# Gate fold spread singly among the tiles of turns 0 and 1, an own bank for y of chunk 1, last sums in two parts, compares in halves with idle products in search 2

## The chip, the cores and the metric

The kernel runs on one core of a Trainium2 chip. The time is device microseconds of one execution. Engines are named as in the profile: PE is TensorE (PEld its weight loads), DVE is VectorE, ACT is ScalarE, POOL is GpSimd, SP is SyncE, whose queue issues most DMAs.

## The reference, cut to what matters

Three stages follow each other, all in float32:

```python
# attention with a decaying state: B, H, S, D = 4, 8, 768, 48
for t in range(S):
    cur = einsum('bhd,bhe->bhde', u[None] * kt, vt)
    y[:, :, t] = einsum('bhd,bhde->bhe', rt, state + cur)
    state = wt[..., None] * state + einsum('bhd,bhe->bhde', kt, vt)
# x = y as 3072 rows of 384
h = x @ w_in                      # 384 -> 2048
g = h * tanh(log1p(exp(h)))
x = g @ w_out                     # 2048 -> 384
# experts, each with room for 384 of the 3072 rows
logits = x @ w_gate               # 8 experts
# the (row, expert) pairs in order of falling logit: a row goes to the first
# expert in its order that is not yet full
for e in range(8):
    out[mask] = maximum(x[mask] @ w1[e], 0) @ w2[e]
```

## The kernel before, in words

**Tiling.** The 3072 rows are 24 chunks of 128 rows. Two chunks make a turn (`CH = 2`), so there are 12 turns. Matrix products run as three float16 products: high part by high part, low by high, high by low. Every engine has its own program, a list in order written out by hand; semaphores join them. What stands ahead of what is fixed by the `turn(i, slot)` functions, 16 slots to a turn.

**The attention of a chunk n.** DVE makes the running product of the decays (`products`), its reciprocal in two parts (`inverse`), `kdiv` (`key_side`, L926) and `rdec` (`query_side`, L933). PE makes the scores (`scores`), DVE masks them (`masks`, into `att`), PE turns kdiv (`keys`) and makes y into a PSUM bank and the state's increment into another (`values`, L440). POOL makes the diagonal products r*k*u (`diagonal`) and dv (`own`), with the dot products of DVE (`dots`) between the two. DVE adds y and dv (`sum_x`, L955), PE turns x (`turn_x`, L467) into the bank of y, ACT rounds it to `x_hi`, DVE makes `x_lo` from it. y of every chunk is in bank 7 (`Y`); `values(n)` therefore waits for x_hi and x_lo of the chunk before. The first two chunks run ahead of turn 0, with idle products (`warm`) on PE in between.

**A turn's slots.** In slots 0 to 7 PE runs the 8 tiles of x @ w_in (`tile(i, j)`, 18 products of 128x256 each, into three banks in rotation). Tile j >= 3 waits for DVE's copy of tile j - 2 (`copied`, L988, semaphore `hcp`), so tile (1,3) waits for the copy of tile (1,0). In slots 8 to 15 PE runs `sums(i - 1, j)`, 12 products of 128x392 each, of the turn before, into banks 0 and 1; turn 0 has none. ACT does tanh and arctan in slots 0 to 8, the sines at slot 8, and rounds g afterwards; DVE multiplies (`gated`, L995) in slots 9 to 15, ahead of the copies of the next turn. The attention of later chunks is laid between the slots; in turn 0 that of chunks 2 and 3, in slots 3 to 7.

**The gate fold.** w_out @ w_gate is made once on PE: 16 column groups of three float32 products of 128x8 each, 48 in all, into bank 0. From there ACT and DVE put it beside w_out as 8 more columns (392 instead of 384), so that the sums give the logits too; these two copies, `foldhi` and `foldlo`, stand in slot 4 of ACT and slot 6 of DVE in turn 1, and `sums(0, 0)` waits for them. The fold runs in four blocks of 12 products: after tile (0,3), at the end of slot 7 of turn 0, and in slots 1 and 2 of turn 1. Its turned weights lie in the buffers of g_hi and g_lo (first two quarters) and in two of their own.

**The end of the first stage.** After the last turn PE makes only the logits of its two chunks (`last_logits`), then two of their eight sums. The other six are laid into search 1.

**The searches.** Expert by expert (7 searches, r = 0 to 6) a threshold is searched in 6 steps of 32 limits. A step: DVE compares 24 columns of keys with 32 limits (`compare`, L1209, 128x768), PE counts (`counts`, 24 products of 8 columns), DVE tests `full`, PE spreads it (`maxima`), DVE reduces it (`most`) and makes the next limits. After 6 steps `choose` names the expert and its rows, `ranks` numbers them, the next search starts. The experts' products are laid between: for expert p, X turns the gathered rows, H0 to H7 are the first product (9 products of 128x384), Y0 to Y7 the second. In search 1 no expert is ready; behind the maxima of each step stands one of the six late sums. In search 2 (r = 1) PE has only units I and J (the row numbers of the first expert, for the gather by POOL), then X in step 4, H0 and H1 in step 5, and H2, Y0, H3 after it. From search 3 on PE is full. Units are placed by this table:

```python
PLACES = {("A", 0): ["Y1"], ("B", 0): ["H4"], ("A", 1): ["I", "Y2"], ("B", 1): ["J", "H5"],
          ("A", 2): ["Y3"], ("B", 2): ["H6"], ("A", 3): ["Y4"], ("B", 3): ["H7"],
          ("A", 4): ["Y5"], ("B", 4): ["X", "Y6"], ("A", 5): ["Y7"],
          ("B", 5): ["H0", "H1"], ("C", 0): ["H2", "Y0", "H3"]}
```

All matrix products are recorded at L413 (the helper `mm`), all activations at L726, so they are told apart by their operands: fold products read `w_gate`, scores `rdec,kdiv`, idle products `ident` alone, counts `oh,cmp`, maxima `full`. A float32 product of PE has two records. The start of PE's program, where `values(1)` stands between `keys(1)` and `turn_x(1)`, is L594 to L611; the searches on PE begin at L617.

Of the kernel before, what the change touches and what calls it, by code (L numbers as in the profile page):

```python
# [13 lines left out]
P = 128  # L14
# [45 lines left out]
def moe_chain(nc, wt_d, kt_d, rt_d, r_d, k_d, v_d, u_d, win_d, wout_d, wg_d, wot_d, w1_d, w2_d, out_d):  # L60
# [4 lines left out]
    with ctx:  # L65
# [3 lines left out]
        def sem(name):  # L69
# [129 lines left out]
                 "oh", "cmp", "cnt", "full", "np", "mem", "rank", "numbered", "one_hot", "copies", "idblk", "blocks", "idps", "ids", "maxin", "maxout", "rd",  # L199
# [41 lines left out]
        STEPS = 2  # L241

# [168 lines left out]
        def _(pe):  # L411
# [28 lines left out]
            def values(n):  # L440
# [4 lines left out]
                pe.wait_ge(s["xhi"], n)  # L445
                pe.wait_ge(s["xlo"], n)
                pe.wait_ge(ld["v"][c], 16 * (n // CH + 1))
                for q in range(NQ):
                    if not first_of(n):
                        mm(Y[:, 2 * q * D:(2 * q + 2) * D], rdec[c][:, q, :], state[:, q, :], start=True, stop=False)  # L450
                    for h in (2 * q, 2 * q + 1):
                        last = mm(Y[:, h * D:(h + 1) * D], att[:, h, :], v_tok[c][:, h, :],
                                  start=first_of(n), stop=first_of(n) or h % 2 == 1)
# [9 lines left out]
            def turn_x(n):  # L463
                c = n % CH
                pe.wait_ge(s["x"], n + 1)
                for k3 in range(KT):
                    last = nc.tensor.transpose(Y[:, k3 * P:(k3 + 1) * P], x_tok[c][:, k3 * P:(k3 + 1) * P],  # L467
                                               ident[:, :])
                last.then_inc(s["xT"], 1)

            def tile(i, j):
# [13 lines left out]
                elif i == 0:  # L485
                    pe.wait_ge(s["att"], 4)
                for f in range(2):
# [28 lines left out]
            def sums(i, j):  # L516
# [9 lines left out]
                rounded_parts(i, j)  # L526
                for c in range(CH):
                    for f in range(2):
                        t = (2 * j + f) * TOK + c * P
                        hi_, lo_ = g_hi[:, t:t + P], g_lo[:, t:t + P]  # L530
                        first, end = j == 0 and f == 0, j == NJ - 1 and f == 1
                        mm(ab[c][:, 0:DE], hi_, wout_hi[:, 2 * j + f, :], start=first, stop=False)
                        mm(ab[c][:, 0:DE], hi_, wout_lo[:, 2 * j + f, :], start=False, stop=False)
                        last = mm(ab[c][:, 0:DE], lo_, wout_hi[:, 2 * j + f, :], start=False, stop=end)
                last.then_inc(s["mm"], 1)
# [3 lines left out]

            def folded(qs):  # L540
                pe.wait_ge(s["gload"], 16)
# [1036 lines left out]
```

## Time and profile before

| | us |
|---|---|
| median of 3 runs | 848.12 |
| lowest, highest | 845.80, 849.88 |
| the profiled execution: its time | 849.38 |
| the profiled execution: its span | 847.6 |
| PE busy in it | 802.7 |
| DVE busy in it | 641.2 |
| ACT busy in it | 405.4 |
| POOL busy in it | 282.4 |

The span is the time from the first to the last instruction of the profiled execution; all instants below count from its start. The mean granted clock of PE is 0.968 of full speed. Busy PE includes the modelled ends of pipelined products, so it hides short gaps. The stages by time: the first two chunks up to 30 us, turn 0 to 67, turn 1 with the sums of turn 0 to about 118, the other turns to 556, search 1 to 587, search 2 to 614, five more searches with the experts, then the last experts alone.

### The profile page before, as it was taken

Reading aid. Unit: us, or ns where it says so; the run is one execution under the profiler, and the core shown is the slowest. Engines: PE = TensorE matmul, PEld = TensorE weight load, DVE = VectorE, ACT = ScalarE, POOL = GpSimd, SP = SyncE. Lnnn points to the kernel's source line nnn. Section 1 sums busy time; section 2 is a strip of 40 time slices with the busy share of each in tenths; the row PEclk is TensorE's granted clock in tenths of the full one; section 3 lists DMA queues with packets and bytes.
Section 4 is the critical chain, followed back from the end, with each engine's and each line's share of the span. In section 5 each row is a group of like instructions: output and inputs, shape, how many; then the busy total and the mean of one; then the engine's idle time right before and its main releaser. Section 6 shows DMA issues by size and latency. Waiting matters only on the chain. (4 is left out here: it accounts for less than half of the span.)

```text
span 847.6 us, 16953 instructions
## 1 busy us (share of the span) xinstructions
PE 802.7 (95%) x6744; PEld 596.4 (70%) x6744; DVE 641.2 (76%) x1123; ACT 405.4 (48%) x655; POOL 282.4 (33%) x244
## 2 busy tenths in 40 slices
PE   8999999999999999999898999986799999999995
PEld 8888878787878787868676777754465665666662
DVE  8879788898979897979696987767768677776220
ACT  2457557575767667575756476920112211212221
POOL 3315262534444443444251625001212312313311
PEclk9897999999999999999999999998599999999999
DMA  9952236363545445463817354103324244235410
GB/s 312 334 193 61 72 125 249 105 243 125 218 155 201 173 168 207 140 232 120 315 59 289 121 182 136 75 20 131 139 106 177 68 167 178 89 146 205 190 43 29
DMA packets 47790, 133.48 MB, mean 157 GB/s; under 512 B 5344, under 2 KB 19808, under 8 KB 45664
## 3 DMA queue, kind: packets, MB, share of 16 engines
q1 hardware_dynamic: 38880, 93.07, 31.2%
q0 software_dynamic: 5376, 34.61, 11.1%
q10 hardware_dynamic: 3456, 4.72, 1.5%
q8 instruction: 54, 0.88, 0.4%
q14 instruction: 24, 0.20, 0.1%
HBM read 97.78 MB, written 34.60 MB: 156 GB/s over the span
## 5 line engine op out<-in xcount | busy, mean ns | idle before, releaser
L413 PE MATMUL bank<-x_hi,win_hi 128*128 128x256 f16 x576 | 160.5, 279 | 0.0
L413 PE MATMUL bank<-x_lo,win_hi 128*128 128x256 f16 x576 | 160.3, 278 | 0.0
L413 PE MATMUL bank<-x_hi,win_lo 128*128 128x256 f16 x576 | 160.1, 278 | 0.0
L1438 POOL TENSOR_TENSOR g_lo<-t_sb,g_hi 128x512 f16<-128x512 f32 x88 | 117.4, 1355 | 82.0 <-ACT g_hi L726 82.0
L413 PE MATMUL bank<-wout_hi,g_hi 128*128 128x392 f16 (+1 forms) x416 | 129.5, 318 | 0.8 <-issue 0.8
L413 PE MATMUL bank<-wout_lo,g_hi 128*128 128x392 f16 (+1 forms) x416 | 129.2, 317 | 0.0
L413 PE MATMUL bank<-wout_hi,g_lo 128*128 128x392 f16 (+1 forms) x416 | 129.1, 317 | 0.0
L1422 POOL TENSOR_TENSOR dv<-v_tok,dot 128x384 f32<-128x384 f32 x24 | 39.6, 1649 | 210.3 <-DVE dot L948 210.3
L726 ACT ACTIVATE g_lo<-bank 128x384 f16<-128x384 f32 x64 | 31.4, 490 | 144.5 <-PE bank L413 144.5
L726 ACT ACTIVATE g_hi<-t_sb 128x512 f16<-128x512 f32 x96 | 56.8, 624 | 89.1 <-DVE t_sb L995 65.9
L995 DVE TENSOR_TENSOR t_sb<-t_sb,h_sb 128x512 f32<-128x512 f32 x96 | 89.8, 964 | 5.4 <-ACT t_sb L726 3.4
L726 ACT ACTIVATE t_sb<-h_sb 128x512 f32<-128x512 f32 x96 | 60.1, 626 | 64.5 <-DVE h_sb L988 64.4
L918 DVE RECIPROCAL inv<-cum 128x256 f32<-128x256 f32 x48 | 83.3, 1737 | 0.0
L988 DVE TENSOR_SCALAR h_sb<-bank 128x512 f32<-128x512 f32 x96 | 64.0, 667 | 15.9 <-PE bank L413 15.9
L726 ACT ACTIVATE t_sb<-t_sb,half 128x512 f32<-128x512 f32 x96 | 67.1, 706 | 0.0
L1309 DVE SCALAR_TENSOR_TENSOR g_lo<-bank,g_lo 128x384 f16<-128x384 f32 x64 | 35.1, 549 | 41.0 <-ACT g_lo L726 40.6
L413 PEld LDWEIGHTS bank<-x_hi,win_hi 128*128 128x128 f16 x576 | 58.3, 101 | 9.3 <-issue 0.2
L413 PEld LDWEIGHTS bank<-x_lo,win_hi 128*128 128x128 f16 x576 | 57.5, 100 | 7.9
L413 PEld LDWEIGHTS bank<-x_hi,win_lo 128*128 128x128 f16 x576 | 57.6, 100 | 7.7
L726 ACT ACTIVATE stage<-stage 128x1536 f16<-128x1536 f32 (+1 forms) x33 | 48.6, 1473 | 25.5 <-DMA stage<-in_moe_w 25.5
L726 ACT ACTIVATE t_sb<-t_sb,half_pi 128x512 f32<-128x512 f32 x96 | 60.7, 709 | 0.1
L413 PEld LDWEIGHTS bank<-wout_hi,g_lo 128*128 128x128 f16 x416 | 40.1, 98 | 26.4 <-issue 0.3
(179 smaller groups left out, 1514.0 us busy)
## 6 DMA issues: line engine op xcount, KB each, us to landing
stage<-in_moe_w SPq DMA_DIRECT2D x32, 768.0 KB, 6.7
w_split<-stage SPq DMA_DIRECT2D x32, 768.0 KB, 5.3
wt<-in_w_turned SPq DMA_DIRECT2D x24, 258.0 KB, 5.3
kt<-in_k_turned SPq DMA_DIRECT2D x24, 256.0 KB, 4.8
rt<-in_r_turned SPq DMA_DIRECT2D x24, 256.0 KB, 5.2
r_tok<-in_r SPq DMA_DIRECT2D x24, 192.0 KB, 6.5
k_tok<-in_k SPq DMA_DIRECT2D x24, 192.0 KB, 6.8
v_tok<-in_v SPq DMA_DIRECT2D x24, 192.0 KB, 4.8
```

Of the source, the lines that this page charges most:

```text
L413: return nc.tensor.matmul(*a, **k)
L726: return nc.scalar.activation(out, in_, f, **k)
L918: V.reciprocal(inv[:, qs, :], cum[n % CH][:, qs, 1:PW]).then_inc(s["inv"], 1)
L988: V.tensor_scalar(h_sb[:, j * GW:(j + 1) * GW], hb[HB[j]][:, :], 0.5, None, ALU.mult).then_inc(s["hcp"], 1)
L995: V.tensor_tensor(t, t, h_sb[:, j * GW:(j + 1) * GW], ALU.mult).then_inc(s["g"], 1)
L1309: V.scalar_tensor_tensor(h_lo[f % 3][:, :], bank[3 + f % 3][:, 0:CAP], 0.0, h_hi[f % 3][:, :], ALU.max, ALU.subtract).then_inc(s["hlo"], 1)
L1422: G.tensor_tensor(dv[:, :, :], v_tok[c][:, :, :], dot[:, :].rearrange("p (h o) -> p h o", o=1).to_broadcast([P, H, D]), ALU.mult).then_inc ...
L1438: G.tensor_tensor(g_lo[:, j * GW:(j + 1) * GW], t_sb[:, j * GW:(j + 1) * GW], g_hi[:, j * GW:(j + 1) * GW], ALU.subtract).then_inc(s["glo" ...
```

## The change

Five edits, of which the diff shows the core. (1) y, its turned x and their readers use bank 1 for chunk 1 alone, and the values of chunk 1 no longer wait for x_hi and x_lo of chunk 0; three idle products stand ahead of them. POOL waits for rdec of chunk 1 before its diagonal. (2) The 48 fold products are issued one at a time behind every third product of a tile: six in each of tiles 4 to 7 of turn 0, four in each of tiles 0 to 5 of turn 1; the wait for their weights stands ahead of tile (0,4). ACT's copy of the gate columns moves from slot 4 to 6, DVE's from 6 to 7. (3) Of each of the six late sums in search 1, 3 of 12 products now stand ahead of the maxima and 9 behind. (4) In searches 1 and 2 the compare is two instructions of half the columns, and the counts begin on the first half. (5) In search 2 PE gets idle products (float32, 128 columns, into a bank not in use): 14 before it, 4 after the first counts, 5 after each of the maxima of steps 0 to 3. 

```diff
+        def y_bank(n):
+            return ab[1] if n == 1 else Y
...
                 pe.wait_ge(s["att"], 2 * n + 2)
                 if not first_of(n):
                     pe.wait_ge(s["state"], with_keys(n))
-                pe.wait_ge(s["xhi"], n)
-                pe.wait_ge(s["xlo"], n)
+                if n > 1:
+                    pe.wait_ge(s["xhi"], n)
+                    pe.wait_ge(s["xlo"], n)
                 pe.wait_ge(ld["v"][c], 16 * (n // CH + 1))
...
+            to_fold = [(t, k3) for t in range(FT) for k3 in range(KT)]
+            FOLDS = {**{(0, j): 6 for j in range(4, NJ)}, **{(1, j): 4 for j in range(6)}}
+
+            def fold_one():
+                t, k3 = to_fold.pop(0)
+                q, f = t // (FT // 4), t % (FT // 4)
+                last = mm(ab[0][:, t * E:(t + 1) * E], wot[q][:, k3, f * P:(f + 1) * P], w_gate[:, k3, :],
+                          start=k3 == 0, stop=k3 == KT - 1)
+                if f == FT // 4 - 1 and k3 == KT - 1:
+                    last.then_inc(s["fold"], 1)
...
+                folds = FOLDS.get((i, j), 0)
+                if (i, j) == (0, 4):
+                    pe.wait_ge(s["gload"], 16)
+                    pe.wait_ge(s["wotload"], 64)
...
                         last = mm(hb[HB[j]][:, f * TOK:(f + 1) * TOK], a, b, start=t == 0, stop=t == len(ops) - 1)
+                        if folds and t % 3 == 1 and 3 * f + t // 3 < folds:
+                            fold_one()
...
                     if slot == 3:
-                        folded([0])
                         scores(2)
...
                         turn_x(3)
-                        folded([1])
...
-                if i == 1 and slot in (1, 2):
-                    folded([slot + 1])
...
             keys(1)
+            warm(ident[:, :], 3)
             values(1)
...
-                pe.wait_ge(s["cmp"], NSTEP * r + t + 1)
+                if r < 2:
+                    pe.wait_ge(s["cmp_half"], NSTEP * r + t + 1)
+                else:
+                    pe.wait_ge(s["cmp"], NSTEP * r + t + 1)
                 for j in range(NT):
+                    if r < 2 and j == NT // 2:
+                        pe.wait_ge(s["cmp"], NSTEP * r + t + 1)
                     last = mm(R[0:NTHR, 0:E], cmp[:, j, :], oh[:, j, :], start=j == 0, stop=j == NT - 1)
...
+            def idle_products(n):
+                for _ in range(n):
+                    mm(yb[2][:, 0:P], ident[:, :], ident[:, :], start=True, stop=True)
+
             for r in range(E - 1):
+                if r == 1:
+                    idle_products(14)
                 for t in range(NSTEP):
                     counts(r, t)
+                    if r == 1 and t == 0:
+                        idle_products(4)
                     units(r, ("A", t), unit)
+                    if r == 0:
+                        sums(NI - 1, SUMS["B", t], slice(0, 3))
                     maxima(r, t)
+                    if r == 1 and t < 4:
+                        idle_products(5)
                     units(r, ("B", t), unit)
                     if r == 0:
-                        sums(NI - 1, SUMS["B", t])
+                        sums(NI - 1, SUMS["B", t], slice(3, None))
...
-                if i == 1 and slot == 4:
+                if i == 1 and slot == 6:
                     act.wait_ge(s["fold"], 4)
...
-                    if i == 1 and slot == 6:
+                    if i == 1 and slot == 7:
                         dve.wait_ge(s["foldhi"], 1)
...
+            def compare(x, limits, parts):
+                n = NT // parts
+                for h in range(parts):
+                    x_part = x[:, h * n:(h + 1) * n].rearrange("p (j o) -> p j o", o=1).to_broadcast([P, n, NTHR])
+                    ins = V.tensor_tensor(cmp[:, h * n:(h + 1) * n, :], x_part,
+                                          limits[:, :].rearrange("p (o i) -> p o i", o=1).to_broadcast([P, n, NTHR]),
+                                          ALU.is_ge)
+                    ins.then_inc(s["cmp" if h == parts - 1 else "cmp_half"], 1)
...
             own(0)
+            pool.wait_ge(s["rdec"], 2)
             diagonal(1)
             own(1)
```

## Rows read from the trace of the kernel before

**Rows 1.** Table of stretches; PEclk is the granted clock, each engine busy us (xcount).

```profile
24.60:31.40 6.80, 6.80 (x35) 6.30 (x34) 4.51 (x8) 3.34 (x3) 2.24 (x3) 0.50 1.03 413
...
41.70:45.10 3.40, 3.40 (x21) 2.81 (x20) 2.83 (x4) 3.25 (x5) 0.00 (x0) 0.50 0.77 246
...
65.60:86.00 20.40, 20.40 (x129) 16.54 (x128) 17.83 (x18) 14.33 (x23) 12.58 (x10) 0.67 0.18 53
...
588.00:600.00 12.00, 4.43 (x107) 3.65 (x107) 9.33 (x32) 0.00 (x0) 2.97 (x3) 0.50 0.69 272
```

**Rows 2.** Timeline, PE, start of the kernel: start, us, engine, line, operation, idle before.

```profile
15.53 2.87 PE L413 MATMUL bank<-ident 128*128 128x128 f32 x24
...
22.30 0.43 PE L413 MATMUL bank<-state,rdec 128*128 128x96 f32 x2 [0.94 <-DVE x_lo L981]
...
29.88 0.42 PE L413 MATMUL bank<-x_hi,win_hi 128*128 128x256 f16 x1
```

**Rows 3.** Timeline, POOL and DVE, chunk 1 ahead of turn 0.

```profile
16.73 1.34 POOL L1415 TENSOR_TENSOR ruk<-ruk,u_b 128x384 f32<-128x384 f32 x1
...
17.12 1.49 DVE L933 TENSOR_TENSOR rdec<-rt,cum 128x512 f32<-128x512 f32 x1
...
25.56 0.56 DVE L955 TENSOR_TENSOR x_tok<-bank,dv 128x384 f32<-128x384 f32 x1 [1.40 <-PE bank L413]
```

**Rows 4.** Timeline, PE, turn 0: a fold block, tile (0,6) to what follows it, scores.

```profile
38.50 2.74 PE L413 MATMUL bank<-w_gate,g_hi 128*128 128x8 f32 x24
...
52.32 0.27 PE L413 MATMUL bank<-x_hi,win_hi 128*128 128x256 f16 x1
...
54.29 0.49 PE L467 MATMUL bank<-ident,x_tok 128*128 128x128 f32 x3
...
55.43 1.68 PE L413 MATMUL bank<-rdec,kdiv 64*128 64x128 f32 x16 [0.65 <-DVE kdiv L926]
```

**Rows 5.** Timeline, DVE, turns 0 and 1.

```profile
38.00 0.69 DVE L933 TENSOR_TENSOR rdec<-rt,cum 128x512 f32<-128x512 f32 x1
...
62.46 0.56 DVE L955 TENSOR_TENSOR x_tok<-bank,dv 128x384 f32<-128x384 f32 x1 [0.51 <-PE bank L413]
...
67.01 3.76 DVE L995 TENSOR_TENSOR t_sb<-t_sb,h_sb 128x512 f32<-128x512 f32 x6 [1.43 <-ACT t_sb L726]
...
78.22 0.68 DVE L988 TENSOR_SCALAR h_sb<-bank 128x512 f32<-128x512 f32 x1
```

**Rows 6.** Timeline, DVE and PE, searches 1 and 2.

```profile
566.20 0.96 DVE L1209 TENSOR_TENSOR cmp<-key,thr 128x768 bf16<-128x768 f32 x1
...
565.51 0.17 PE L413 MATMUL bank<-full,rest_b 32*128 32x8 bf16 x1 [0.68 <-DVE full L1219]
...
567.71 0.76 PE L413 MATMUL bank<-oh,cmp 128*32 128x8 bf16 x24
...
568.78 0.17 PE L413 MATMUL bank<-full,rest_b 32*128 32x8 bf16 x1 [0.32 <-DVE full L1219]
...
588.40 0.78 PE L413 MATMUL bank<-oh,cmp 128*32 128x8 bf16 x24 [4.00 <-DVE cmp L1209]
...
588.59 0.46 DVE L1281 TENSOR_TENSOR t_sb<-high,iota_hi 128x288 f16<-128x288 f32 x1
...
592.25 0.80 PE L413 MATMUL bank<-oh,cmp 128*32 128x8 bf16 x24 [1.54 <-DVE cmp L1209]
...
595.10 0.80 PE L413 MATMUL bank<-oh,cmp 128*32 128x8 bf16 x24 [1.10 <-DVE cmp L1209]
...
595.96 0.17 DVE L1303 TENSOR_SCALAR ids<-row_no 128x3 uint32<-128x3 f32 x1
```

**Rows 7.** Timeline, PE, end of search 2 and first counts of search 3.

```profile
602.28 2.18 PE L659 MATMUL bank<-ident,h_sb 128*128 128x128 f32 x9 [0.17 <-DMA h_sb<-x_rows,ids]
...
605.81 5.94 PE L413 MATMUL bank<-g_hi,win_hi 128*128 128x384 f16 x18
...
616.15 0.76 PE L413 MATMUL bank<-oh,cmp 128*32 128x8 bf16 x24
```

More of the change, by code:

```diff
@@ L198, in moe_chain @@
                  "phi", "plo",
-                 "oh", "cmp", "cnt", "full", "np", "mem", "rank", "numbered", "one_hot", "copies", "idblk", "blocks", "idps", "ids", "maxin", "maxout", "rd",
+                 "oh", "cmp", "cmp_half", "cnt", "full", "np", "mem", "rank", "numbered", "one_hot", "copies", "idblk", "blocks", "idps", "ids", "maxin", "maxout", "rd",
                  "wrow", "xg", "xgT", "xgThi", "xgTlo", "hh", "hhi", "hlo", "m2", "ylast", "y", "yout"]
@@ L514, in last_logits, with sums @@
                 last.then_inc(s["logit"], 1)
-            def sums(i, j):
+            def sums(i, j, part=slice(0, None)):
                 if i == 0 and j % 2 == 0:
@@ L526, in sums @@
                 rounded_parts(i, j)
+                ops = []
                 for c in range(CH):
@@ L530, in sums @@
                         hi_, lo_ = g_hi[:, t:t + P], g_lo[:, t:t + P]
+                        w_hi, w_lo = wout_hi[:, 2 * j + f, :], wout_lo[:, 2 * j + f, :]
                         first, end = j == 0 and f == 0, j == NJ - 1 and f == 1
[L532 to L535, printed above, removed]
+                        ops += [(c, hi_, w_hi, first, False), (c, hi_, w_lo, False, False), (c, lo_, w_hi, False, end)]
+                for c, g, w, start, stop in ops[part]:
+                    last = mm(ab[c][:, 0:DE], g, w, start=start, stop=stop)
+                if part.stop is None:
+                    last.then_inc(s["mm"], 1)
             def finish(i, step):
                 pass
-            def folded(qs):
-                pe.wait_ge(s["gload"], 16)
-                pe.wait_ge(s["wotload"], 64)
-                for q in qs:
-                    for f in range(FT // 4):
-                        t = q * FT // 4 + f
-                        for k3 in range(KT):
-                            last = mm(ab[0][:, t * E:(t + 1) * E], wot[q][:, k3, f * P:(f + 1) * P], w_gate[:, k3, :],
-                                      start=k3 == 0, stop=k3 == KT - 1)
-                    last.then_inc(s["fold"], 1)
             def turn(i, slot):
@@ L1227, in next_step @@
                                                 ALU.mult, ALU.add))
-                    compare(key, thr)
+                    compare(key, thr, 2 if r < 2 else 1)
                     link(V.scalar_tensor_tensor(lo[t + 1][:, :], m, w, lo[t][:, :], ALU.mult, ALU.add))
@@ L1236, in next_step @@
                     link(V.tensor_scalar(res[:, :], near[:, :], lo[t + 1][:, 0:1], None, ALU.subtract))
-                    compare(res, grid[NSTEP - 1])
+                    compare(res, grid[NSTEP - 1], 2 if r < 2 else 1)
             def weight_row(r, x):
@@ L1368, in _ @@
                 if r < E - 2:
-                    start_search()
+                    start_search(r + 1)
                     digits()
```

23 lines of the change are left out of this document (10 added, 13 removed).

## The prediction

> **What bounds the kernel now.** I began with the page: TensorE is busy for 802.7 of 847.6 us, so time can only come from its idle stretches, its half-clock stretches and its work. The table of stretches then shows where the clock falls [rows 1]: 0.50 is the level of 1.2 GHz, 1.00 that of 2.4 GHz. It is 0.50 from 24.6 to 31.4 us, from 41.7 to 45.1, on average 0.67 from 65.6 to 86.0 (three spells, 13.5 us at half), 0.50 from 588 to 600, and the products that follow run at that pace too [rows 7]. These are the stretches that the change touches. The timelines say what lay ahead of each fall: at the start a wait and narrow float32 products [rows 2]; in turns 0 and 1 a block of gate folds [rows 4]; in search 2 an almost idle TensorE [rows 6]. Between turn 2 and the end of the sums TensorE has no gap that the edits touch, so I let every microsecond won before it arrive at the end.
>
> **The start.** Chunk 1's values wait 0.94 us for x_lo of chunk 0 [rows 2]. With a bank of its own for y that goes, and three idle products stand there, at 2.87 / 12 = 0.24 us each [rows 2]. The new POOL wait keeps diagonal(1) off VectorE's rdec(1), which took 1.49 us where rdec(2) takes 0.69 [rows 3, 5], while POOL's product ran beside it (16.73 to 18.07) [rows 3]. diagonal(1) then ends near 20.2 instead of 18.1; who waits for it is dots(1), queued behind masks(1), which even in the new order end near 20.8, so the wait costs nothing. Without that cover it costs up to 2.1. scores(1) can start 0.4 us earlier (the 12 idle products ahead of it end at 18.4), y of chunk 1 is done near 24.0, and with TensorE busy throughout I expect full clock there. sum_x(1) then waits for dv(1) (near 24.3), no longer 1.40 us for TensorE [rows 3], and tile (0,0) starts near 27.15 instead of 29.88 [rows 2], at full clock. VectorE's queue (products, split, copies, reciprocals) then ends rdec(2) at 35.6 instead of 38.7 [rows 5]. **Gain 3.1 us.**
>
> **Turn 0 from there.** A tile is 54.29 - 52.32 = 1.97 us; a fold in its block is 2.74 / 12 = 0.22 us, its two weight loads being longer than its 8 columns [rows 4]. Interleaved, a fold costs from 0 (hidden) to about 0.33 (its 0.22 and one more exposed load); I take 0.22, the nearest row. Today rdec(2) to the end of y of chunk 3 is 62.4 - 38.7 = 23.7 us [rows 5]. Afterwards: scores 1.65, a wait of 0.65 for the split of weight piece 2, tiles 4 to 7 with six folds each 4 x (1.97 + 1.34) = 13.2, keys twice 1.0, values(2) 3.6, turn_x 0.45, scores(3) 1.65, y(3) 2.6: 24.8 us. The wait for the gate's weights moves from ahead of 38.50, where it holds up nothing [rows 4], to about 37.9: 0 to 0.6 us, and I take 0. No DMA is moved. The block of 12 after tile 3 and the half clock behind it go, but the second block, which lay behind y(3), now lies ahead of it. **Loss 1.1 us, net gain 2.0.** By bounds of the fold: gain 4.6 or 0.
>
> The Trainium skill, "TensorE: Matmul & The Clock Gate", Step-by-step: what each phase is for, says that weight loads are pulled ahead of running matmuls into the background buffer. By that rule one of a fold's two loads lies under the 256-column product, a fold costs 0.11, and turn 0 would win 2.7 us more.
>
> **Turn 1.** ScalarE's sines and VectorE's gating set the next date: gated products from 67.01 after a wait for ScalarE, then reciprocals, kdiv, rdec, and the copy of tile (1,0) only at 78.22 [rows 5]; tile (1,3) waits for that copy. All this moves up by 2.0, to 76.9. TensorE, at full clock and without blocks, is through tiles 0 to 2 at about 72 (start 63.5, three times 1.97 + 0.88) and idles some 5 us. So most of the 6.7 us that the half clock cost from 65.6 to 86.0 is not won: the stretch turns VectorE-bound. Idle for 4.00 us before 588.40 was followed by half clock [rows 1, 6], so tile (1,3) starts at half clock again. Tile 3 at half clock takes 4.9, scores 1.65, tiles 4 and 5 with their folds 5.7, keys 0.5, tile 6 1.97, values(4) 3.6, tile 7 1.97: 76.9 + 20.3 = 97.2, less 0.4 for what is back at full clock within it, instead of today's 99.5. If the clock holds all along, VectorE's queue sets it, and it is 94.5. The later gate copies (slots 6 and 7) put a wait of up to 1.6 us before sum_x(4), which stands in for one of 1.4 us for TensorE; turn_x(4) comes a tile later, so I cost it at nothing; without that tile it would be 0.5. **Gain up to here 2.7 (2.3 to 5.0).**
>
> **Search 1.** A step is 568.78 - 565.51 = 3.27 us and bound by TensorE: counts 0.76, a wait of 0.32 for `full`, the maxima 0.1, and the 12 sums with the rest, 2.1 [rows 6]. Three sums (0.5 us) now fill that wait and delay the maxima by 0.19, nine stay behind: a step becomes some 2.9 instead of 3.27. Five steps win 0.4 each, 2.0 (1.5 if the sums' own 0.31 is all). The compare in halves lengthens VectorE: 384 elements cost 0.56 us by the line through 288 (0.46) and 768 (0.96) [rows 6], and instructions start 0.08 before the last ends, so 0.08 more each, behind TensorE here except at the first (-0.1). The later maxima before choose costs 0.2, which leaves 1.7. **Gain 1.8**, since the maxima of the first step, where `full` waits for VectorE, move by nothing.
>
> **Search 2.** A step is 595.10 - 592.25 = 2.85 us and VectorE-bound: TensorE waits 1.54 us for the compare [rows 6], then 24 counts. With halves, 12 counts lie under the second half; won 0.38 a step at full clock, none below half that. What matters is the ids at 595.96 [rows 6], two steps in: gather and transposes (which ended their wait on the gather, [rows 7]) start about 2.2 us earlier in all. The 14 idle products (3.3 us at full clock) fit before 588.40, where TensorE waits 4.00 us [rows 6]; the 4 fit before `full`; 5 after the maxima (1.2 us) end as the first half compare does (566.20 - 565.51 = 0.69 from maxima to compare, and its 0.56, [rows 6]). They cost nothing at full clock. Their cover is gone at half clock, where five take 5 x 0.47 = 2.35 us.
>
> The H products behind the transposes ran from 605.81 at half clock, 18 in 5.94 us, and counts of search 3 started at 616.15 [rows 7]. If the clock holds all through, up to 3.0 us come back there and 0.6 in the transposes. But TensorE idles again before the gather lands and before H0, so I take half, 1.5. **Gain of both searches 1.8 + 0.4 + 1.5 = 3.7 (2 to 5.8).**
>
> The Trainium skill, "VectorE: DVE Perf Modes", The TRN2 errata, gives a fixed term of about 150 cycles for each instruction, an estimate of 0.16 us. By that rule each split compare costs 0.16 and not the 0.08 of my line, and the searches win 0.5 us less.
>
> **Sum.** 2.7 + 3.7 = 6.4. The profiled execution took 849.4 us (span 847.6), the median of the runs is 848.1: 843.0 on the first, 841.7 on the second. I forecast 841.7, by the median.
>
> **Rivals.** (A) Forecast, 839 to 843.9: 0.50. (B) The clock holds where I let it fall (tile (1,3), H0): 5.0 + 5.8 = 10.8, 837.3 to 839. For: TensorE keeps far busier; against: both idle stretches stay. 0.20. (C) The idle products don't hold the clock in search 2. A step is then 0.10 + 2.35 + 0.07 + 0.76 + 0.37 = 3.65 instead of 2.85, four cost 3.2, the transposes start 0.9 late: searches lose 0.9 in place of 3.7 won, 848.1 - 2.7 + 0.9 = 846.3. For: the counts between them are only 8 columns wide. Against: float32 products of 128 columns held the clock at the start. 0.12. (D) The start keeps its half-clock spell, or VectorE's queue eats the win in turns 0 and 1: turns give 0.5 to 1.0, 843.5 to 844. 0.12. (E) **Slower:** the folds, a third of the time of their tiles, pull the clock down for whole tiles as the blocks did. Tiles 4 to 7 of turn 0 then take 13.2 us more, tiles 3 to 5 of turn 1 some 5 more beyond the cover: 848 + 18 - 6 = 860. It decides at tile (0,4), where the granted clock would be 0.50. Against: two thirds of each tile stay 256 columns wide. 0.06.
>
> **Numbers.** About 0.5% (4.2 us) is what a measurement of this kernel can tell from no change; the bound is 843.9. Faster is A, B and half of D: 0.76. Same is C and half of D: 0.18. Slower is E: 0.06. The range 837 to 846.5 holds B to C and leaves out E, and the chance that several terms err the same way.
>
> **What would show it.** Right: clock 1.00 from 24 to 31 and 41 to 66; first product of a tile near 27; singles of 8 columns between products of 256, spaced 0.22 more; TensorE idle 4 to 5 us before tile (1,3), waiting for `h_sb`; search 1 steps of 2.9; search 2 steps of 2.5 and ids near 593.8 less the turns' 2.7. Wrong: half clock in a tile with folds; folds spaced beyond 0.33; tile (1,3) without a wait; search 2 steps above 2.85.

## The result, and the profile after

The changed kernel took 852.33 us (median of 6 runs, 850.13 to 852.88) against 848.04 (6 runs, 845.61 to 849.88) of the kernel before on the same chip: a ratio of 1.004, 95% interval 1.0021 to 1.0059. The forecast was 841.7, in a range of 837 to 846.5. A second measurement with more runs, `after_again` below, is 1.0025. The change is a small loss, and the prediction was wrong in size and sign. The profiled execution took 852.56 us, its span is 850.8 (before 847.6).

The ledger below has the start of the same VectorE or TensorE work in the two profiled executions (`late` is a VectorE instruction that stands once, at the end of a search).

| | before | after | difference |
|---|---|---|---|
| tile (0,0), first product | 29.88 | 27.90 | -1.98 |
| rdec(2) | 38.00 | 38.64 | +0.64 |
| x_tok(3), end of turn 0 | 62.46 | 65.01 | +2.55 |
| x_tok(4), turn 1 | 96.77 | 98.51 | +1.74 |
| x_tok(5) | 110.32 | 111.08 | +0.76 |
| `full` of search 1, first step | 565.29 | 566.21 | +0.92 |
| `late`, end of search 1 | 582.24 | 582.04 | -0.20 |
| `late`, end of search 2 | 606.12 | 609.93 | +3.81 |
| `late`, end of search 3 | 639.82 | 643.05 | +3.23 |

In these two executions, then, two things went wrong: between 28 and 39 us the whole gain of the start is lost, and search 2 costs 4.0 us. From search 3 on the two run in step.

One execution stands for each side, and the kernel before varies much by itself, since its half clock does not always fall in the same place. `searchonly`, an experiment below, is the kernel before up to search 1, and its profile has x_tok(5) 4.20 us earlier than the 110.32 of the ledger:

```profile
106.12 0.56 DVE L965 TENSOR_TENSOR x_tok<-bank,dv 128x384 f32<-128x384 f32 x1 [0.36 <-PE bank L413]
```

`beforewait`, the kernel before with one more wait, has it at 108.11. A difference of some 4 us up to search 1 in such a ledger is thus no gain or loss of a kernel; the medians decide that.

**28 to 39 us.** The timelines of VectorE and GpSimd of the changed kernel (start, us, engine, line, operation, idle before):

```profile
27.53 1.44 DVE L940 TENSOR_TENSOR_SCAN cum<-wt,heads 128x516 f32<-128x516 f32 x1
28.89 4.64 DVE L1038 SCALAR_TENSOR_TENSOR win_lo<-stage,win_hi 128x1536 f16<-128x1536 f32 x1
33.46 0.68 DVE L1019 TENSOR_SCALAR h_sb<-bank 128x512 f32<-128x512 f32 x1
...
38.64 0.68 DVE L964 TENSOR_TENSOR rdec<-rt,cum 128x512 f32<-128x512 f32 x1
```

```profile
28.83 3.09 POOL L1466 TENSOR_TENSOR win_lo<-stage,win_hi 128x1536 f16<-128x1536 f32 x1 [0.95 <-ACT win_hi L757]
```

VectorE's split of a weight piece took 4.64 us. The same kind of split takes 1.75 at 21.64 in this profile. GpSimd's split of another piece had begun 0.06 us earlier; it ended at 28.83 + 3.09 = 31.92, and VectorE's ended 1.61 later, about its own length. VectorE's queue is 2.9 us late from there, and TensorE with it:

```profile
27.90 0.27 PE L416 MATMUL bank<-x_hi,win_hi 128*128 128x256 f16 x1 [1.44 <-DVE x_lo L1012]
...
33.64 0.27 PE L416 MATMUL bank<-x_hi,win_hi 128*128 128x256 f16 x1 [1.65 <-issue]
...
39.42 1.75 PE L416 MATMUL bank<-rdec,kdiv 64*128 64x128 f32 x16 [1.70 <-DVE kdiv L957]
```

Tile (0,0) does start 1.98 us earlier, but two waits of 1.65 and 1.70 us follow which the kernel before does not have there, and half clock comes after them, just where the tiles carry their folds. The table of stretches (us, then each engine's busy time, then PEclk) shows this and the other half-clock stretches:

```profile
24.60:31.40 6.80, 5.36 (x48) 4.66 (x48) 6.61 (x8) 3.35 (x3) 4.62 (x3) 1.00 1.04 409
40.90:47.60 6.70, 6.19 (x36) 5.14 (x36) 4.50 (x7) 3.75 (x5) 2.48 (x3) 0.50 0.70 237
68.40:71.70 3.30, 3.30 (x22) 2.85 (x21) 2.26 (x4) 3.29 (x6) 0.00 (x0) 0.51 0.05 18
81.90:85.90 4.00, 4.00 (x24) 3.18 (x23) 4.00 (x5) 1.58 (x4) 4.00 (x3) 0.58 0.43 132
...
590.70:609.00 18.30, 16.50 (x180) 14.74 (x180) 11.24 (x40) 1.47 (x3) 3.16 (x3) 0.50 0.36 136
```

The first row answers to the first of [rows 1]: full clock at the start, as forecast. But 6.7 us at half in turn 0 stand where 3.4 were. The last row lies within a stretch at half from 590.4 to 614.3; in the kernel before it was from 587.8 to 611.7, as long. So the idle products did not hold the clock here, they only stood in a stretch that was at half before too.

**The folds.** TensorE in tile (0,6), a fold after each third product, and what follows the tile:

```profile
54.09 0.27 PE L416 MATMUL bank<-x_hi,win_hi 128*128 128x256 f16 x1
54.20 0.27 PE L416 MATMUL bank<-x_lo,win_hi 128*128 128x256 f16 x1
54.31 0.29 PE L416 MATMUL bank<-w_gate,g_lo 128*128 128x8 f32 x2
54.45 0.27 PE L416 MATMUL bank<-x_hi,win_lo 128*128 128x256 f16 x1
...
56.89 0.49 PE L472 MATMUL bank<-ident,x_tok 128*128 128x128 f32 x3
```

The tile is 56.89 - 54.09 = 2.80 us instead of 1.97 [rows 4], so six folds cost 0.83, **0.14 apiece**; in a block they cost 0.22.

**Turn 1 and search 2.** TensorE ahead of tile (1,3), and in search 2:

```profile
81.37 0.28 PE L416 MATMUL bank<-x_hi,win_hi 128*128 128x256 f16 x1 [3.93 <-DVE h_sb L1019]
...
590.53 2.50 PE L416 MATMUL bank<-ident 128*128 128x128 f32 x10
592.96 0.80 PE L416 MATMUL bank<-oh,cmp 128*32 128x8 bf16 x24
...
597.84 2.50 PE L416 MATMUL bank<-ident 128*128 128x128 f32 x10
600.27 0.80 PE L416 MATMUL bank<-oh,cmp 128*32 128x8 bf16 x24
...
609.62 5.40 PE L416 MATMUL bank<-g_hi,win_hi 128*128 128x384 f16 x18
```

Five idle products take 2.50 us at half clock, and the counts stand behind them without a wait: VectorE's compares are done 0.8 us before them (at 592.14 for the counts at 592.96). A step takes 3.67 us (590.21 to 593.88 by `full`), the next 3.63, 4.58 and 3.67, where they took 2.83 to 2.88 before [rows 6]. In the step of 4.58 VectorE's `full` also started 0.9 us later after the counts than in the others, which the profile before has nowhere (see Open).

### The profile page after: what moved, and what is told of

Same layout as the page of the kernel before. It is cut to its first block and busy times, and to the rows that moved or that the text cites. A ratio compares the mean times of both kernels' runs of the same rounds, so it can differ in the third digit from the quotient of the medians.

```text
span 850.8 us, 17130 instructions
## 1 busy us (share of the span) xinstructions
PE 809.4 (95%) x6826; PEld 602.4 (71%) x6826; DVE 644.6 (76%) x1135; ACT 405.6 (48%) x655; POOL 281.1 (33%) x244
## 5 line engine op out<-in xcount | busy, mean ns | idle before, releaser
L757 ACT ACTIVATE g_lo<-bank 128x384 f16<-128x384 f32 x64 | 31.4, 491 | 143.9 <-PE bank L416 138.7
L1026 DVE TENSOR_TENSOR t_sb<-t_sb,h_sb 128x512 f32<-128x512 f32 x96 | 90.4, 971 | 5.4 <-ACT t_sb L757 3.4
L416 PEld LDWEIGHTS bank<-x_hi,win_lo 128*128 128x128 f16 x576 | 62.0, 108 | 6.0
```

Source lines behind the costliest of these rows:

```text
L416: return nc.tensor.matmul(*a, **k)
L757: return nc.scalar.activation(out, in_, f, **k)
L1026: V.tensor_tensor(t, t, h_sb[:, j * GW:(j + 1) * GW], ALU.mult).then_inc(s["g"], 1)
```

## The experiments

Each ratio is to the kernel before, run beside it on the same chip. Its own median moved from chip to chip (848.23, 849.25, 846.05 and 846.02 us), so ratios are compared, and medians only where both kernels ran on one chip.

### The two suspects: `poolwait`, `noidle`, `both`, `foldonly`

`poolwait` makes GpSimd's splits wait until VectorE's second split of this kind is done; `noidle` takes out the idle products of search 2; `both` does both.

```diff
             def split_scaled(n):
                 pool.wait_ge(s["whi"], n + 1)
+                pool.wait_ge(s["wlo"], 2)
...
             for r in range(E - 1):
-                if r == 1:
-                    idle_products(14)
...
-                    if r == 1 and t == 0:
-                        idle_products(4)
...
-                    if r == 1 and t < 4:
-                        idle_products(5)
```

`foldonly` is the kernel before with the second edit alone: folds spread, gate copies later.

> The changed kernel plus one wait: POOL's win_lo (weight piece 3) waits until VectorE's split of piece 1 is done. Theory P (the win at the start is lost because POOL's product started at 28.83, 0.06 us before VectorE's split, which then took 4.64 us instead of 1.73): VectorE's split takes 1.7 again, rdec of chunk 2 ends near 36.4 instead of 39.3, the first masks and x_tok of turns 0 and 1 come 2.5 to 3 us earlier, and the whole is 2 to 3 us faster than the changed kernel, near 849.5. Rival (the stretch is bound elsewhere, by the fold or by weights from HBM): no more than 0.5 us comes back.

> The changed kernel without the 14, 4 and 5 idle products of search 2; all else kept. Theory I (the idle products fell to half clock and stood in front of the counts): the steps of search 2 go back to 2.6 to 2.85 us, search 2 loses nothing against the kernel before, the whole is 4 to 5 us faster than the changed kernel, near 847.5. Rival (the loss in search 2 comes from the halves): steps stay near 3.7 and nothing comes back.

> The POOL wait and no idle products together. If both theories hold and the two add, 6.5 to 8 us faster than the changed kernel: near 845, 3 us faster than the kernel before. If one hides the other, less than 5.

> The kernel before with the fold spread alone (and the later gate copies that go with it). Own theory (fold costs 0.14 us apiece between wide products and keeps the clock; turn 1 is VectorE-bound all the same): 1 to 2 us faster than the kernel before, near 846.5, with an idle wait of some 4 us ahead of tile (1,3). Rival (the spread fold is itself what costs 0.8 us by turn 2): 0.5 to 1.5 us slower.

| | median, us (range, runs) | ratio, 95% |
|---|---|---|
| poolwait | 848.36 (845.31 to 854.31, 12) | 1.0005, 0.9981 to 1.0029 |
| noidle | 849.96 (847.41 to 855.16) | 1.0031, 1.0011 to 1.005 |
| both | 845.67 (843.54 to 849.8) | 0.9973, 0.9954 to 0.9992 |
| foldonly | 851.69 (846.85 to 856.28, and one of 2777.86) | 1.0033, 1.0007 to 1.0059 |

**The splits.** VectorE's and GpSimd's split in `noidle`, in `poolwait` and in `foldonly`, a fence for each view:

```profile
29.16 1.73 DVE L1032 SCALAR_TENSOR_TENSOR win_lo<-stage,win_hi 128x1536 f16<-128x1536 f32 x1
```

```profile
29.32 4.53 POOL L1460 TENSOR_TENSOR win_lo<-stage,win_hi 128x1536 f16<-128x1536 f32 x1 [2.02 <-ACT win_hi L751]
```

```profile
29.34 1.73 DVE L1038 SCALAR_TENSOR_TENSOR win_lo<-stage,win_hi 128x1536 f16<-128x1536 f32 x1
```

```profile
31.21 3.10 POOL L1467 TENSOR_TENSOR win_lo<-stage,win_hi 128x1536 f16<-128x1536 f32 x1 [3.74 <-DVE win_lo L1038]
```

```profile
29.45 4.65 DVE L1009 SCALAR_TENSOR_TENSOR win_lo<-stage,win_hi 128x1536 f16<-128x1536 f32 x1
```

```profile
29.39 3.10 POOL L1432 TENSOR_TENSOR win_lo<-stage,win_hi 128x1536 f16<-128x1536 f32 x1 [1.81 <-ACT win_hi L728]
```

Whoever starts first takes its own time, and the other's ends one full length behind it: in `noidle` 29.16 + 1.73 = 30.89, and GpSimd's ends at 33.85, 2.96 later. In `foldonly`, which has the old start, GpSimd was first by 0.06 us. Of the eight profiled executions of this study without the added wait VectorE's split took 4.6 us in four (the changed kernel in all three of its profiles, and `foldonly`). In the other four it took 1.7 and GpSimd's 3.7 to 4.6. The Trainium skill, "SBUF — State Buffer", Who interferes with whom, says that a VectorE instruction with two SBUF inputs contends with a GpSimd instruction that reads SBUF, that the shared pair of ports is locked by one of them, and that the order of issue decides who blocks. Every one of these rows agrees. With the wait, x_tok(2) starts at 49.34 in `poolwait` instead of 53.36.

**Search 2.** In `poolwait` the same code had full clock until 602.4 us and its steps took 2.56, 2.93, 3.97 and 3.20; in `noidle` the clock was at half, and they took 2.59, 2.95, 3.86 and 2.60. At half clock, then, the change's idle products cost 0.7 to 1.1 us a step, 3.6 over the whole of search 2 (27.9 us against 24.3 in `noidle`). From `late` of search 1 to that of search 3 `noidle` wins 0.7 us on the kernel before, the changed kernel loses 3.4. In the medians the difference of `both` to `poolwait` is 2.7 us (the idle products; the intervals just overlap), that of `noidle` to the changed kernel's own measurement 2.4 (on another chip, 0.8 by ratios). `both` and `noidle` ran on one chip and differ in GpSimd's wait alone: 4.3 us, and the intervals lie apart. This is the test of the collision in the medians. It is more than the 3 us of one collision, and in the one profiled execution of `noidle` VectorE's split happened to come first, so what else the wait changes isn't known. Neither cause alone explains the loss; with both taken out the kernel is 0.27% faster than before, still not the 0.76% of the forecast.

### Turn 1: `bothfill`, `earlyfill`, `startonly`, `searchonly`

In `both` TensorE still idles 3.94 us ahead of tile (1,3), and half clock follows (76.8 to 80.2); in `poolwait` it lasted from 76.7 to 90.4. `bothfill` fills 3.74 us of that wait. `earlyfill` has 9 products there and the folds of turn 1 eight to a tile in tiles (1,0) to (1,2). `startonly` and `searchonly` are the kernel before with edit (1), or with (3) and (4), alone.

```diff
             def tile(i, j):
...
+                if (i, j) == (1, 3):
+                    for _ in range(16):
+                        mm(ab[1][:, 0:P], ident[:, :], ident[:, :], start=True, stop=True)
                 if j >= 3:
                     pe.wait_ge(s["hcp"], NJ * i + j - 2)
```

> The POOL wait and no idle products in search 2, plus 16 idle float32 products (3.8 us at full clock, into bank 1) ahead of tile (1,3), where TensorE waits for VectorE's copy of tile (1,0). Theory T (turn 1's half clock comes from that wait, and the folds in tiles (1,3) to (1,5) then keep it): the granted clock stays 1.00 from 66 to 100 us, x_tok of chunks 4 and 5 come at least as early as in the best profile so far (93.4 and 106.0), and the slow executions of the kernel without the fill (848 to 850) go: median 843 to 844.5. Rival (the clock falls whatever TensorE does in the wait): half clock stays, nothing gained, or up to 2 us lost because 16 products at half clock outlast the wait.

> As the last, but turn 1's 24 folds stand 8 to a tile in tiles (1,0) to (1,2), ahead of the wait, and 9 idle products fill what is left of it. Theory T: the folds cost nothing there, since TensorE would wait anyway; tiles (1,3) to (1,5) take 1.97 us each; 1 to 1.7 us faster than the kernel with 16 idle products if TensorE bounds the rest of turn 1, equal to it if VectorE does. Rival (folds belong among busy tiles): the clock falls in tiles (1,0) to (1,2), where folds take 1.1 of 3.1 us.

> The kernel before with the start's edits alone (own y bank for chunk 1, three idle products, POOL behind rdec). Theory P: the tile (0,0) starts 2 us earlier, VectorE's split of weight piece 1 meets POOL's win_lo again and takes 4.6 us in most executions, so that nothing is left by x_tok of chunk 2: within 1 us of the kernel before. Rival: the start's win stays, 2 to 3 us faster.

> The kernel before with the late sums in two parts and the compares in halves alone, no idle products. By the steps in the profiles so far: search 1 gains 1.2 us, search 2 at half clock about 0.3 net; 1 to 2 us faster than the kernel before, near 846.7. Rival (the halves cost more on VectorE than they hide): same or slower.

| | median, us (range) | ratio, 95% |
|---|---|---|
| bothfill | 843.63 (841.82 to 844.67) | 0.9938, 0.9919 to 0.9958 |
| earlyfill | 843.1 (841.98 to 846.21) | 0.9944, 0.9924 to 0.9964 |
| startonly | 847.89 (843.45 to 850.32) | 0.9986, 0.9962 to 1.0009 |
| searchonly | 846.95 (842.6 to 849.86) | 0.9976, 0.9953 to 0.9998 |

`bothfill` and `earlyfill` had full clock from 14 to 100 us, and their executions lie within 2.9 and 4.2 us of each other where those of `both` lie within 6.3: the slower executions are gone, as they would be if the clock had stayed down in these (only one execution of each was profiled). x_tok(5) is 4.57 us earlier than in the profile before in `bothfill`, 5.06 in `earlyfill`, but only 0.37 and 0.86 earlier than in `searchonly`, so the ratios and not this must carry the gain. The two do not differ in time. Against the 0.9973 of `both` the fill is worth 0.35%; by `bothfill_again` below (0.9951) it is 0.2%, with intervals that overlap. The start alone can't be told from nothing, though in its profile VectorE's split came first and took 1.7. The edits of the searches alone win 0.24%, with the upper end of the interval at 0.9998.

### The idle products of search 2: `allfill`, `hold`, and two controls

`allfill` is the changed kernel, idle products in, with the wait of GpSimd and the fill. `hold` is `earlyfill` with its idle products behind the counts, where they delay none of the step's work: 14 ahead, 7, 1, 1, 1, 1 and 4 behind the counts of the six steps, 5 behind the units of steps 0 to 3, 6 ahead of the transposes. `beforewait` is the kernel before with GpSimd's wait; `after_look` is one more execution of the changed kernel.

```diff
                     counts(r, t)
-                    if r == 1 and t == 0:
-                        idle_products(4)
+                    if r == 1:
+                        idle_products((7, 1, 1, 1, 1, 4)[t])
...
+                    if r == 1 and t == 4:
+                        idle_products(6)
                     units(r, ("B", t), unit)
```

> The changed kernel with all its idle products in search 2, the POOL wait and 16 idle products ahead of tile (1,3). The stages up to the sums are then as in the kernel with both fills and no idle products in search 2 (843.6), so the difference is the price of search 2's idle products alone. Theory I: they fall to half clock in most executions and cost 2 to 4 us: median 846 to 847.5, and executions spread more. Rival (they keep the clock more often than not when the stages before are steady): no dearer than 0.5 us, or up to 2 us faster.

> The kernel with early folds and fill (843.1), with more idle products in search 2, placed behind units I and J instead of ahead: 14 ahead of it, 7 after the first counts, 1 after those of steps 1 to 4, 5 behind the units of steps 0 to 3, 6 ahead of the transposes, 4 after the last counts. Theory H (the clock of search 2 can be held if no gap of TensorE is left, and H0 to H2 then run at full clock): granted clock 1.00 from 560 to 620, search 2 3 to 4 us shorter, median 839.5 to 840.5. Rival (the clock falls all the same and the idle products then stand in front at half clock): 3 to 5 us slower, 846 to 848.

> The kernel before with the POOL wait alone. In three other profiles with the old start TensorE kept its clock there, and POOL's win_lo and VectorE's split of piece 1 then start within 0.3 us of each other. Theory P (whoever comes second waits, and it is a toss in the kernel before too): the executions in which VectorE loses go, 0.5 to 2 us faster in the median. Rival (only the changed kernel has the meeting): no difference.

> The changed kernel once more, to see what of its profile is the kernel's and what the execution's. Theory: the meeting of POOL and VectorE at 29 us is a toss (4.6 or 1.7 us for VectorE's split), the idle wait ahead of tile (1,3) is there each time, and half clock in search 2 begins at another place. Rival: all three as in the first profile.

`allfill` 842.71 us (838.75 to 846.74), ratio 0.9957 (0.994 to 0.9973); `hold` 843.5 (841.86 to 845.01), 0.9959 (0.9945 to 0.9974); `beforewait` 846.76, 1.0002 (0.9985 to 1.0019); `after_look` 847.25 in its one execution. In `allfill` and `hold` the granted clock was 1.00 through all of search 2, and from `late` of search 1 to that of search 3 they won 3.5 and 2.4 us on the kernel before. `after_look` had it until 602.9, with steps of 2.55, 2.94, 2.54 and 2.56 us, by the same code that took 3.67, 3.63, 4.58 and 3.67. So the clock was up through the idle products' steps in some executions of this code and down in others. Of the five profiled executions that have them it fell at 590.4 us in the changed kernel's first, between 602 and 609 in three, and not at all in `allfill`; only the first was at half through the steps that hold idle products. And `allfill` keeps all five edits: with GpSimd's wait and the fill the changed kernel is 0.43% faster than the one before, so the idle products are not what makes it a loss. GpSimd's wait is worth nothing to the kernel before. `hold` had half clock from 64.1 to 81.1 us, through its tiles with eight folds; the same tiles had full clock in `earlyfill`.

### What was still open: `after_again`, `foldfill`, `best`, `bothfill_again`

`foldfill` is `foldonly` with GpSimd's wait and the fill. `best` is `bothfill` with the idle products of `hold`.

> The changed kernel once more, beside the kernel before on the same chip. Theory: its loss is made of two stretches, each of which goes one way or the other: the splits of weights near 29 us (VectorE's takes 4.6 us where GpSimd's starts first: about 2 us late up to tile (1,3), partly covered by the wait there) and search 2 (steps of 3.6 to 4.6 us if the half clock comes before its counts, 2.55 if it doesn't: 4 us). So 1.000 to 1.005 of the kernel before; in the profile, VectorE's copy near 28.9 us takes 4.6 us, and TensorE waits near 4 us before tile (1,3). Rival (the first measurement was a matter of its chip): 0.996 or less.

> The kernel before with the fold spread singly and the gate copies late, plus the wait of GpSimd's split and 16 idle products ahead of tile (1,3). Without those two it was 1.0033. Theory (the spread folds cost 0.14 us each and win only if the clock stays up through the tiles that carry them): 0.995 to 0.998, no half clock from the end of tile (1,2) to turn 2. Rival (spreading wins nothing whatever the clock does, since the folds only move): 1.000 or more.

> The changed kernel with the wait of GpSimd's split, 16 idle products ahead of tile (1,3), folds four to a tile in turn 1, and in search 2 idle products placed as in the run named hold (7, 1, 1, 1, 1, 4 behind the counts of the six steps, 6 ahead of the transposes). Theory (turn 1 with four folds a tile keeps full clock, eight a tile did not in hold; search 2 keeps it with products after the counts): 0.991 to 0.994, granted clock 1.00 from 60 to 100 us and from 585 to 615. Rival (idle products in search 2 win nothing over none): 0.994 to 0.997, as with the kernels that had none there or had them ahead of the counts.

> The run named bothfill again (wait of GpSimd's split, 16 idle products ahead of tile (1,3), none in search 2), beside the last one on the same chip, for the price of idle products in search 2 alone. Theory (they hold the clock there): bothfill is 0.5 to 2.5 us slower than the last one. Rival (they win nothing): equal within 0.5 us, near 0.994 of the kernel before.

| | median, us (range, runs) | ratio, 95% |
|---|---|---|
| after_again | 849.17 (844.44 to 853.43, and one of 2753.59; 12) | 1.0025, 1.0003 to 1.0046 |
| foldfill | 843.97 (842.48 to 846.73, 12) | 0.9965, 0.9949 to 0.998 |
| best | 841.86 (840.56 to 847.31, 12) | 0.9951, 0.9933 to 0.9969 |
| bothfill_again | 842.45 (840.64 to 844.09, 10) | 0.9951, 0.9933 to 0.9969 |

**The loss is the kernel's**, not the first chip's: 1.0025 here. Its profile has the long split again (29.44, 4.58 us) and TensorE waits 5.53 us ahead of tile (1,3), with half clock from 79.9 to 93.6 us around its end and behind it: x_tok(3) is 1.83 us later than before, x_tok(4) 4.51. In search 2 the clock held, and it won 0.8 us there.

**Spreading the folds** together with the fill and GpSimd's wait wins 0.35%, and alone (`foldonly`) it loses 0.33%: the same 48 products. The profile of `foldonly` has both troubles, the long split and a stretch at half clock from 78.2 to 88.4; that of `foldfill` has neither. The wait alone won nothing in `beforewait`; the fill was not tried without the spread folds, so what spreading by itself is worth isn't shown.

**Idle products in search 2** are worth nothing measurable: `best` and `bothfill_again` have the same ratio, though in the profiles `best` kept full clock and won 2.35 us from `late` of search 1 to that of search 3, `bothfill_again` at half clock 0.96. Two stretches of `best`, then the first product of an expert in it:

```profile
66.00:100.00 34.00, 31.14 (x287) 27.55 (x286) 31.90 (x38) 20.72 (x35) 17.87 (x13) 1.00 0.23 69
588.00:600.00 12.00, 11.72 (x169) 10.51 (x167) 9.15 (x33) 1.25 (x3) 3.03 (x3) 1.00 0.37 129
```

```profile
600.85 3.10 PE L416 MATMUL bank<-g_hi,win_hi 128*128 128x384 f16 x18
```

The 18 products of H0 and H1 take 3.10 us there against 5.40 in the changed kernel and 5.94 before [rows 7]. But `best` was 1.9 us behind `bothfill_again` when search 1 began, where the two have the same code. It had half clock from 458.1 to 461.5 and from 553.7 to 557.1 us, in the last logits (some 0.7 us of the 1.9), and `bothfill_again` had none there. The same two stretches come and go among the other profiles too; what decides it was not tried.

## Why the prediction was wrong

**The step that failed** in every profile of the changed kernel is the last one of the start: "VectorE's queue (products, split, copies, reciprocals) then ends rdec(2) at 35.6". I took that queue's durations from a profile in which GpSimd's split of 3.72 us began 0.97 us after VectorE's of 1.73, and moved VectorE's forward by 1.6 us without asking where GpSimd's would land. It landed 0.06 us ahead, and rdec(2) came at 38.64. I had even priced the same collision elsewhere, at rdec(1). rdec(2) ended at 39.3, and at 39.8 in the other two profiles. With the same start and GpSimd held back it ends at 36.3 (in `bothfill_again`) to 36.9 in seven profiles, and at 38.1 in `poolwait`, which had half clock from 28.9 to 32.3. Of the 3.7 us by which that step was wrong 2.4 to 3.0 are the collision.

**Two more steps failed with it.** "They cost nothing at full clock", of the idle products in search 2, was right as it stands, but full clock did not last: at half clock they cost 3.6 us in the first profile and nothing in the other two. And "tile (1,3) starts at half clock again" was given one tile, where it lasted up to 17 us. With GpSimd's wait and the fill added, and nothing taken out, the ratio goes from 1.0025 or 1.0040 to 0.9957 (`allfill`).

- *The start.* Full clock: right in the first profile; in `after_again`, `after_look` and `poolwait` it was at half from about 29 to 32.5. Tile (0,0) at 27.15: it came at 27.90 (its x_lo started at 27.05), and at 28.6 in the two later profiles. rdec(1) took 0.69 us instead of 1.49, as GpSimd's new wait was meant to bring. But the 3.1 us of gain were counted against an execution with half clock from 24.6 to 31.4. Of the five profiles with the old start only that one and `foldfill` have it. In `searchonly`, with the old start and full clock there, tile (0,0) came at 28.58 and rdec(2) ended at 36.9:

```profile
24.60:31.40 6.80, 5.42 (x50) 4.97 (x49) 6.07 (x9) 3.35 (x3) 3.82 (x3) 1.00 1.03 411
```

  Against such an execution a rdec(2) that ends at 36.3 wins 0.6 us, which fits `startonly`, whose gain can't be told from nothing. To take that half clock for the kernel's own was part of the error.
- *A fold costs 0.22.* It cost 0.14, between my row and the 0.11 by the rule of the Trainium skill, "TensorE: Matmul & The Clock Gate", Step-by-step: what each phase is for; 24 of them in turn 0 win 1.9 us more. (The upper bound "gain 4.6" belongs to 0.11; for a hidden fold it would be 2.0 + 24 x 0.22 = 7.3.) At half clock this is lost again: 6.7 us at half instead of none cost some 3.4 there, an estimate, behind waits that the late rdec(2) made. With neither (`bothfill`), x_tok(3) is 2.39 us earlier than in the profile before, the forecast 2.0. That is in part luck: in `searchonly` the old code has it 2.04 earlier.
- *Turn 1.* "Idles some 5 us" before tile (1,3): 3.93, right in kind, and 5.53 in `after_again`. "Starts at half clock again": right, but I let it last one tile. Seven profiles have the spread folds and no fill. In `poolwait`, `noidle` and `after_again` half clock lasted 13.7, 17.0 and 13.7 us, through tiles that carry folds, in `foldonly` 10.2, in the other three (the changed kernel's first profile, `after_look`, `both`) 3.4, 6.8 and 3.4. The four long ones stand at waits of 5.5 us and the three short ones at waits of 3.9, here `noidle` and `both`:

```profile
76.42 0.39 PE L416 MATMUL bank<-x_hi,win_hi 128*128 128x256 f16 x1 [5.54 <-DVE h_sb L1013]
```

```profile
76.25 0.28 PE L416 MATMUL bank<-x_hi,win_hi 128*128 128x256 f16 x1 [3.94 <-DVE h_sb L1013]
```

  The three short ones had 3.4 us of half clock in tiles (1,0) and (1,1) as well, so TensorE came later to a wait whose end VectorE sets. Rival E, for which I had given 0.06, had the clock down in all the tiles with folds. What the record shows is that it can stay down through them after a wait; whether the folds keep it down, or the longer wait does, isn't shown, since the same tiles came back after 3.4 us in two profiles.
- *Search 1: gain 1.8.* A step is 3.00 us, not 2.9; 1.1 won by the ledger, 1.1 to 1.3 in the other profiles with the edits. It is the one gain that every profile shows. The split compare was no part of that. In the changed kernel's timeline of VectorE both halves together take 1.02 us against 0.96 of the whole [rows 6]:

```profile
591.12 1.02 DVE L1244 TENSOR_TENSOR cmp<-key,thr 128x384 bf16<-128x384 f32 x2
```

  That is 0.06 for the split, nearer my 0.08 than the estimate of 0.16 worked out from the Trainium skill, "VectorE: DVE Perf Modes", The TRN2 errata.
- *Search 2: gain 1.9.* Lost 4.0 in the first profile, 0.9 of it from one late start of `full` that the profile before lacks; then 0.6 came back. In `after_again` and `after_look` search 2 won 0.8 and 0.9. Rival C had the mechanism and its price (3.65 us a step; 3.67, 3.63 and 3.67 measured, and one of 4.58), with a chance of 0.12. I argued that idle products had held the clock at the start; there they ran without gaps, here they stand between waits of 0.4 to 0.7 us and counts 8 columns wide.
- *Where the clock holds*, in `best`, the searches won 3.7 us on the profile before. That is the forecast's figure, but by luck: the forecast took half of what full clock should give, and by its terms for a clock that holds throughout it was 5.8. x_tok(5) came 4.58 us earlier where those terms gave 5.0, but 4.20 of it are seen in `searchonly` without the edits. In the medians `best` won 0.49%, not 0.76%.

The rivals were weighed one at a time. C and D came together in the first profile, as nothing kept them apart: each is a cover (TensorE without a gap, GpSimd behind VectorE) that the sum assumed. By the ledger the turns lost 0.9 up to search 1 where 2.7 were to be won, and the searches lost 2.3 where 3.7 were to be won: 3.6 and 6.0 of the 9.6 us between the forecast for the profiled execution (843.0) and its 852.6.

**Open.** In step 3 of searches 2 to 7 VectorE's `full` started 0.9 to 1.5 us after the counts had ended, where 0.1 is usual. This was so in the changed kernel's first profile and in every kernel profiled on two of the chips, and in none on the two others or in the profile before; it is part of the 4.58 among the steps. The kernel before had a median of 848.2 and 849.3 us on the first two chips and of 846.0 on the others, but that this is the reason was not tested. What decides whether the clock falls at a given place in one execution and not in the next stayed open. Nor was it found why one execution each of `foldonly` and `after_again` took over 2750 us.

## What to carry to other kernels

When a change moves one engine's queue forward, lay the other engines' long instructions beside it at their new times: here the 0.06 us by which GpSimd's split came first cost VectorE's 2.9. An order that matters should be a semaphore, not a lead of 1 us. Narrow products between wide ones won here only together with a filled wait ahead of them, so look for that wait. Five idle products took 1.38 us at full clock (`after_look`, at 589.53) and 2.50 at half, and delayed what stood behind them, so place them where they delay nothing. And when a gain is a stretch of half clock that goes away, profile the old kernel more than once first: here that stretch was in two profiles of five.

## What was not expected of the hardware

- A float32 product of 8 columns with its two weight loads takes 0.14 us between products of 256 columns, against 0.22 among its own kind.
- At tiles with four products of 8 columns among 18 of 256 TensorE stayed at 1.2 GHz for 10.2 to 17.0 us around and behind a wait of 5.5 us in four profiles, while the same tiles came back after 3.4 to 6.8 us in the three profiles with a wait of 3.9. With 16 idle products of 128 columns (3.74 us) in the wait the level stayed at 2.4 GHz from there to turn 2 in `bothfill`, `bothfill_again`, `allfill`, `foldfill` and `best`, and with 9 in `earlyfill`, though up to 1.97 us of the wait were left.
- The same kernel's clock in search 2 fell at 590.4 us in one execution and at 602.9 or 609.0 in others, and the first took 4.8 to 4.9 us longer over this search.
- The same code's half clock at the start (24.6 to 31.4 us) was there in two of five profiles with the old order, and x_tok(5) of one and the same code came at 110.32 and at 106.12 us.
